# A fused attention and expert kernel: the mixing steps of the last two pairs, the order of the last copies, and the place of the gates

## The chip, the cores and the metric

The kernel runs on one core of one Trainium2 chip. The metric is the device time of the whole program in microseconds, as the median of several runs. The engines are TensorE (PE, with its weight loads PEld), VectorE (DVE), ScalarE (ACT), GpSimd (POOL) and SyncE (SP, which only issues transfers here). They work side by side and are held together by semaphores.

## The reference

Three layers, one behind the other, all in fp32:

```
attention, B=4 batches, H=8 heads, S=576 rows, D=64:
  scores = q @ k.T / 8, causal;  local = softmax(scores) @ v
  phi(x) = elu(x) + 1
  mem    = phi(q) @ M_prev / (phi(q) @ z_prev + 1e-6)
  out    = g * mem + (1 - g) * local,   g = sigmoid(beta) by head
x = out as [2304, 512]
expert layer, 8 experts, F=1024:
  e = argmax(x @ w_gate); gate_w = softmax(x @ w_gate)[e]
  eom = sigmoid(x @ w_output_gate)[e]
  x = gate_w * eom * (relu(x @ w1[e]) @ w2[e])
last layer, 2048 wide:
  h = x @ w_in;  out = (h - tanh(h)) @ w_out
```

## The kernel before, in words

**Attention.** Two heads make a pair; there are NP = 16 pairs (4 to a batch), numbered n from 0. The 576 rows of a pair are QT = 5 steps i of 128 rows (the last has 64). Step m = 5n + i. All engines walk the same two loops, `for n in range(NP + 2)` and `for i in range(QT)`, written out without a loop on the chip, and each has its own order of helpers in the body. For a step, PE computes the scores (`score`), DVE the row maximum (`top`), ACT the exponentials (`exps`), PE turns them (`turn`), and DVE and ACT copy the turned halves to SBUF (`move_a`, `move_b`).

When a pair's five steps are turned, its value products follow one pass later: `average` writes the result for rows 128 to 575 into the PSUM bank `average` (`o_ps[0]`), and `average_first` that for the first 128 into the last quarter of the bank `mix` (`o_ps[1]`, also called `m_ps`). DVE (`move_first`, L880) and ACT (`move_av`, L626) copy both to `ot_sb`. Then come five mixing steps. In `back(n, i)` PE writes phi(q) times M and z, and the turned average, into one bank; in `mix(n, i)` DVE scales both parts to `mixed` (two buffers) with three operations (L897, L900, L905); in `add(n, i)` POOL adds them into `x_sb` (L499) and raises `x_ok`. `phis(n)` on DVE (L911) makes phi(q), `weights_l(n)` (L886 to L891) the sums of the softmax. The banks of the mixing steps are `o_ps[1]`, `o_ps[0]`, `o_ps[1]`, `o_ps[0]`, `o_ps[1]` for i = 0 to 4, so `back` waits from step 2 on for the mix two steps before, and `average` of the next pair waits for `mixed_dve` at 5n - 1, `average_first` at 5n.

**Routing.** When the four pairs of a batch are done, PE turns its `x_sb` (`turn_x`, L1216), ACT copies it (`xlt`), PE makes the logits (`logit`, L1223), DVE picks the expert (`take_logits`, `pick`), PE counts the ranks (`count`), DVE makes row numbers (`place_rows`, `rows_of`), and POOL scatters the rows into `x_sorted` (`scatter`, L506). For batches 0 to 2 this lies inside the passes of the following batch. For the last batch it follows the attention: PE turns step 0 in pass n = 16 between `back(15, 2)` and `back(15, 3)`, step 1 behind `back(15, 3)`, the others behind the loop.

POOL's queue is in order. At pass 16 it does `add(14, 4)`, three scatters of batch 2, then `add(15, 0)` to `add(15, 3)`, at pass 17 `add(15, 4)`, then the five scatters of batch 3.

Behind the routing of the last batch DVE writes how many rows each expert has, and SP and ACT fill unused rows with zeros (`fill`, four each, on their queues; ACT's stand ahead of its `route_exps(B - 1, B)`, L652 and L653). DVE computes the slot table (L1033 to L1061, `r_table`), then waits for ACT's exponentials (`r_exp`), runs `gates_of`, eight operations that make each token's gate (L1012 to L1019), and the corrections L1065 to L1071, and raises `r_tails`. POOL waits for `r_tails` and then makes the low parts of the expert weights, in halves of a unit (L538, `part_lo`); a unit is one expert's w1 or w2. PE meanwhile does 60 idle products (L1172) and then works through 25 slots of 128 rows: `turn_in`, `up` (L1398 to L1400), `turn_hid` (L1420), `down` (L1411 to L1413). `up` of a slot waits for both low halves of its expert's w1. `up` of the next slot is issued ahead of `down` of this one.

In the timelines PE instructions carry the bank's name as their output: `scores`, `turned`, `average`, `mix`, `average` also for the expert layer's results.

Of the kernel before, what the change touches and what calls it, by code (L numbers as in the profile page):

```python
# [8 lines left out]
ALU = mybir.AluOpType  # L9
AX = mybir.AxisListType  # L10

P = 128
B, H, S, D = 4, 8, 576, 64
PAIRS = H // 2
QT = -(-S // P)
NP = B * PAIRS
# [43 lines left out]
def build(nc, qt, qt2, kt2, v, mz, beta, wgo, w1, w2, w_in, w_out, out):  # L60
    ctx = ExitStack()
    with ctx:
# [20 lines left out]
        ident = sb("ident", [P, P], F32)  # L83
# [140 lines left out]
        o_ps = [bank("average"), bank("mix")]  # L224
        m_ps = o_ps[1]

        def mix_ps(i):
            return o_ps[0 if i in (1, 3) else 1]

        def mix4(i):  # L230
            return mix_ps(i)[:, 0:4 * (D + 1)].rearrange("p (a d) -> p a d", a=4)


        c_pool, c_pool2, c_dve, c_dma, c_gate = sem("c_pool"), sem("c_pool2"), sem("c_dve"), sem("c_dma"), sem("c_gate")
# [40 lines left out]
            return [o_ps[0], o_ps[1], t_ps[0]][r]  # L275

        VM = 4 * 16
        last_banks = [s_ps[0][0], s_ps[0][1], s_ps[1][0], s_ps[1][1], o_ps[0]]

        def ring_at(k):  # L280
            return RING - 1 - k % RING
# [547 lines left out]
        def _(dve):  # L829
# [52 lines left out]
            def weights_l(n):  # L882

                p, last = n % 2, QT - 1
                dve.wait_ge(exped, 2 * (n + 1) * QT)
                dve.tensor_copy(sums[0:D, p, last, 1:2], sums[D:P, p, last, 0:1]).then_inc(wts_l, 1)  # L886
                dve.wait_ge(wts_l, 3 * n + 1)
                dve.scalar_tensor_tensor(wts[:, p, :, 0:2], sums[:, p, :, :], 1e-9, inv_l[:, n % PAIRS, :, :], ALU.add, ALU.mult
                                         ).then_inc(wts_l, 1)
                dve.wait_ge(wts_l, 3 * n + 2)  # L890
                dve.reciprocal(wts[:, p, :, 0:2], wts[:, p, :, 0:2]).then_inc(wts_l, 1)  # L891

            def mix(n, i):

                t, p, R = n * QT + i, n % 2, rows(i)
                dve.wait_ge(mixed_pe, t + 1)
                dve.scalar_tensor_tensor(wts[0:R, p, i, 2:4], mix4(i)[0:R, 2:4, D], 1e-6, inv_g[0:R, n % PAIRS, :], ALU.add, ALU.mult  # L897
                                         ).then_inc(wts_step, 1)
                dve.wait_ge(wts_step, 2 * t + 1)
                dve.reciprocal(wts[0:R, p, i, 2:4], wts[0:R, p, i, 2:4]).then_inc(wts_step, 1)  # L900
                dve.wait_ge(wts_step, 2 * t + 2)
                dve.wait_ge(wts_l, 3 * n + 3)
                if t >= 2:
                    dve.wait_ge(x_ok, t - 1)
                dve.tensor_tensor(mixed[0:R, t % 2, :, :], mix4(i)[0:R, :, 0:D], wts[0:R, p, i, :, None].to_broadcast([R, 4, D]),  # L905
                                  ALU.mult).then_inc(mixed_dve, 1)

            def phis(n):
# [64 lines left out]
            for n in range(NP + 2):  # L973
                b, half = divmod(n, PAIRS)
                b -= 1
                for i in range(QT):
                    m = n * QT + i
                    if 0 <= b < B - 1 and i == 3 and half == 2:
                        pick(b)
                    if 0 <= b < B - 1 and i == 3 and half == 3:  # L980
                        rows_of(b)
                        count_so_far(b)
                    if m + 1 < NP * QT:
                        top(m + 1)
                    if 0 <= b < B - 1 and i == 2 and half == 2:
                        take_logits(b, m_ps, LOGITS)
                    if 0 <= b < B - 1 and i == 2 and half == 3:
                        place_rows(b, m_ps, RANKS)
                    if i == 0 and n >= 2:
                        mix(n - 2, QT - 1)  # L990
                    if i == 1 and 1 <= n <= NP:
                        move_first(n - 1)
                    if i == 3 and 1 <= n <= NP:
                        mix(n - 1, 0)
                    if i == 4 and 1 <= n <= NP:
                        mix(n - 1, 2)
                    if n < NP:
                        move_a(m)
                    if i == 3 and n < NP:
                        phis(n)  # L1000
                    if i == 3 and 1 <= n <= NP:
                        mix(n - 1, 1)
                    if i == 4 and 1 <= n <= NP:
                        mix(n - 1, 3)
                    if i == 4 and n < NP:
                        weights_l(n)

            def gates_of(a, z):

                a, z = a * QT, z * QT  # L1010
                sum_e, sum_b = sum_g[:, 0, a:z], sum_g[:, 1, a:z]
                rs(dve.tensor_reduce(sum_e, r_e[:, a:z, :], AX.X, ALU.add))  # L1012
                rs(dve.tensor_scalar(sum_e, sum_e, 1e-9, None, ALU.add))
                rs(dve.reciprocal(sum_e, sum_e))
                rs(dve.tensor_scalar(r_b[:, a:z, :], r_b[:, a:z, :], 1.0, None, ALU.add))
                rs(dve.reciprocal(r_b[:, a:z, :], r_b[:, a:z, :]))
                rs(dve.tensor_tensor(r_b[:, a:z, :], r_b[:, a:z, :], hot[:, a + 1:z + 1, :], ALU.mult))
                rs(dve.tensor_reduce(sum_b, r_b[:, a:z, :], AX.X, ALU.add))
                rs(dve.tensor_tensor(gate[:, a:z], sum_e, sum_b, ALU.mult))  # L1019

            dve.wait_ge(r_exp, 2)
            gates_of(0, B - 1)
            take_logits(B - 1, t_ps[1], 0)
            pick(B - 1)
            place_rows(B - 1, t_ps[0], 0)
# [34 lines left out]
            dve.tensor_scalar(ups[:, :], end_e, 2.0, None, ALU.mult)  # L1060
            dve.tensor_scalar(ends[:, :], end_e, 1.0, None, ALU.add).then_inc(r_table, 1)  # L1061
            dve.wait_ge(r_exp, 4)
            gates_of(B - 1, B)
            wide = [P, TILES, E]
            rs(dve.tensor_tensor(hot2[:, :, :], hot[:, 1:TILES + 1, :], gap_e[:, None, :].to_broadcast(wide), ALU.mult))  # L1065
            rs(dve.tensor_reduce(row_f[:, 1, :], hot2[:, :, :], AX.X, ALU.add))
# [97 lines left out]
        def _(pe):  # L1164
            pe.sem_inc(down_done, 1)
            pe.sem_inc(x_turned, XIN)
            mm = pe.matmul
# [105 lines left out]
            def average(n, js):  # L1273

                p = n % 2
                if js[0] == 0:
                    pe.wait_ge(v_in[p], (n // 2 + 1) * VM)
                    pe.wait_ge(moved_a, (n + 1) * QT)
                    pe.wait_ge(moved_b, (n + 1) * QT)
                    if n:  # L1280
                        pe.wait_ge(mixed_dve, n * QT - 1)
                for j in js:
                    for h in range(2):
                        if j == QT - 1:
                            last = mm(o_ps[0][h * D:(h + 1) * D, S - P - D:S - P], v_sb[0:D, p, j, h * D:(h + 1) * D],
                                      pt_last[0:D, p, h, :], start=False, stop=True)
                        else:
                            a = max(P, j * P)
                            last = mm(o_ps[0][h * D:(h + 1) * D, a - P:S - P], v_sb[:, p, j, h * D:(h + 1) * D],  # L1289
                                      pt[:, p, h, j, a:S], start=j == 0, stop=False)  # L1290
                if js[-1] == QT - 1:
                    last.then_inc(av_done, 1)

            def average_first(n):

                p = n % 2
                if n:
                    pe.wait_ge(mixed_dve, n * QT)
                for h in range(2):
                    last = mm(m_ps[h * D:(h + 1) * D, 512 - P:512], v_sb[:, p, 0, h * D:(h + 1) * D], pt[:, p, h, 0, 0:P],  # L1300
                              start=True, stop=True)
                last.then_inc(first_done, 1)

            def back(n, i):

                t, p, R = n * QT + i, n % 2, rows(i)
                if i == 0:
                    pe.wait_ge(phi_ok, n + 1)
                    pe.wait_ge(first_moved, n + 1)
                else:  # L1310
                    pe.wait_ge(av_moved, n + 1)
                    if i >= 2:
                        pe.wait_ge(mixed_dve, t - 1)
                mm(mix_ps(i)[0:R, 2 * (D + 1):4 * (D + 1)], phi[:, p, i * P:i * P + R],
                   mz_sb[:, p, :, :].rearrange("p h d -> p (h d)"), start=True, stop=True)
                pe.transpose(mix4(i)[0:R, 0:2, 0:D], ot_sb[:, i * P:i * P + R], ident[:, :]).then_inc(mixed_pe, 1)

            score(0)
            for n in range(NP + 2):
# [3 lines left out]
                for i in range(QT):  # L1323
# [27 lines left out]
                            back(n - 1, 2)  # L1351
                    if n < NP:
                        turn(m)
                    if n == NP and i == 4:
                        turn_x((B - 1) * QT, last_banks[0])
                    if 1 <= n <= NP:
                        if i == 0:
                            average(n - 1, [0])
# [2 lines left out]
                        if i == 4:  # L1361
                            back(n - 1, 3)
                    if n == NP and i == 4:
                        turn_x((B - 1) * QT + 1, last_banks[1])
                    if routed and half == 0 and i == 4:
                        turn_x(b * QT, s_ps[(m + 1) % 2][1])
                        turn_x(b * QT + 1, s_ps[m % 2][1])
# [2 lines left out]
                    if routed and half == 1 and i == 4:  # L1370
                        pe.wait_ge(xl_act, b * QT + 3)
                        turn_x(b * QT + 3, s_ps[(m + 1) % 2][1])
                        turn_x(b * QT + 4, s_ps[m % 2][1])

            for i in range(QT):
                if i + 2 < QT:
                    turn_x((B - 1) * QT + i + 2, last_banks[i + 2])
                pe.wait_ge(xl_act, (B - 1) * QT + i + 1)
                logit(i, i % 4, t_ps[1], i * 2 * E).then_inc(logit_ok, 1)
# [153 lines left out]
```

## Time and profile before

| | |
|---|---|
| median of 3 runs | 1031.01 us (1029.05 to 1031.02) |
| profiled execution | 1033.97 us |
| its span in the trace | 1032.1 us |
| mean granted clock of PE | 0.982 of full |
| attention and routing of batches | about 0 to 285 us |
| expert slots | about 300 to 590 us |
| last layer | to the end |

The profile is of one execution. A time in it is counted from the start of the span; an engine's row gives the start and the duration, and in brackets how long the engine had stood idle before, and which engine and line released it ("issue" where the trace shows no releaser). A chain of waits is followed backwards from the last instruction. The column for the granted clock gives PE's clock as a share of 2.4 GHz; 0.50 is 1.2 GHz. The rows themselves stand in a section of their own below.

### The profile page before, as it was taken

The page shows a single profiled execution, that of the slowest core. Times are in us where ns is not written, and L with a number is a line of the kernel's source. Part 1 is how long each engine was busy: PE and PEld are TensorE (multiplying, and loading weights), DVE is VectorE, ACT ScalarE, POOL GpSimd, SP SyncE. Part 2 cuts the span into 40 slices and gives each one's busy share as a digit, 9 for nine tenths or more (in the row PEclk, how much of TensorE's full clock was granted, in tenths as well). Part 3 has the DMA queues.
Part 4 walks back from the last instruction along what each step waited for, and adds up shares of the span by engine and source line. Part 5 has one row for each costly group of instructions (what it writes and reads, how often), then busy time and mean ns, then how long its engine had stood idle before and what let it go on. Part 6 is the DMA issues. An engine that isn't in the chain of part 4 may idle for free.

```text
span 1032.1 us, 16788 instructions
## 1 busy us (share of the span) xinstructions
PE 998.1 (97%) x5474; PEld 821.3 (80%) x5475; DVE 649.1 (63%) x1244; ACT 501.9 (49%) x1043; POOL 468.8 (45%) x332
## 2 busy tenths in 40 slices
PE   6999999899899999999999999999999999999998
PEld 3667667676647888888888879999999999999997
DVE  4687686867544444444444448777777777777764
ACT  5777677686224211022112046556565555555553
POOL 3565587685379933047536137332232322322221
PEclk8999999999889999999999999999999999999999
DMA  9465566531378433146473211010010010100000
GB/s 210 120 164 161 156 191 173 145 108 39 128 250 295 175 123 125 48 150 220 169 273 133 71 41 32 1 31 32 1 62 1 13 50 1 31 31 1 32 1 31
DMA packets 51009, 103.66 MB, mean 100 GB/s; under 512 B 7424, under 2 KB 16640, under 8 KB 50432
## 3 DMA queue, kind: packets, MB, share of 16 engines
q1 hardware_dynamic: 34176, 55.96, 18.8%
q10 hardware_dynamic: 13856, 37.42, 10.2%
q0 software_dynamic: 2912, 9.44, 3.0%
q8 instruction: 37, 0.61, 0.2%
q14 instruction: 28, 0.23, 0.1%
HBM read 82.62 MB, written 20.19 MB: 100 GB/s over the span
## 4 chain that ended last, share of the span: by engine, by line
PE 84%; DVE 10%; issue 2%; POOL 2%; DMA 1%; ACT 1%; ACTq 0%; SPq 0%; DVEq 0%
PE scores L1457 6%; PE scores L1459 6%; PE scores L1458 6%; PE average L1413 4%; PE average L1412 4%; PE average L1411 4%; PE scores L1400 4%; PE scores L1398 4%; PE scores L1399 4%; PE average L1289 4%; PE average L1474 2%; PE scores L1193 2%; PE mix L1475 2%; PE turned L1474 2%; PE average L1475 2%; PE turned L1475 2%
## 5 line engine op out<-in xcount | busy, mean ns | idle before, releaser
L575 POOL TENSOR_TENSOR g_lo<-g,g_hi 128x384 fp32r<-128x384 f32 x96 | 97.9, 1020 | 273.7 <-ACT g_hi L784 273.1
L538 POOL TENSOR_TENSOR ring<-ring 128x2048 fp32r<-128x2048 f32 x30 | 137.4, 4610 | 104.6 <-ACT ring L723 100.8
L723 ACT ACTIVATE ring<-ring 128x2048 fp32r<-128x2048 f32 x30 | 55.7, 1907 | 178.5 <-PE scores L1400 81.7
L1457 PE MATMUL scores<-yt_hi,w_in_hi 128*128 128x384 f32 x384 | 130.9, 341 | 1.7 <-DVE yt_lo L1145 1.7
L1459 PE MATMUL scores<-yt_hi,w_in_lo 128*128 128x384 f32 x384 | 129.3, 337 | 0.0
L1458 PE MATMUL scores<-yt_lo,w_in_hi 128*128 128x384 f32 x384 | 128.8, 335 | 0.0
L774 ACT ACTIVATE sq<-scores 128x384 f32<-128x384 f32 x96 | 47.2, 491 | 163.8 <-PE scores L1459 163.8
L1137 DVE COPY_PREDICATED ser<-big,th 128x384 f32<-128x384 int32 x96 | 119.0, 1240 | 3.3
L1132 DVE TENSOR_TENSOR ser<-ser,sq 128x384 f32<-128x384 f32 x96 | 55.9, 582 | 95.8 <-ACT ser L777 95.8
L601 ACT ACTIVATE prob<-scores,nmx 128x128 f32<-128x128 f32 (+3 forms) x128 | 66.4, 525 | 46.5 <-DVE nmx L862 41.2
L1398 PE MATMUL scores<-ring,xt_hi 128*128 x200 | 80.9, 404 | 3.6 <-POOL ring L538 1.8
L1101 DVE COPY y_sb<-average 128x512 f32<-128x512 f32 x25 | 17.3, 692 | 101.2 <-PE average L1413 101.2
L1411 PE MATMUL average<-ring,hidt_hi 128*128 x200 | 80.0, 400 | 0.6 <-DVE hidt_lo L1095 0.6
L1400 PE MATMUL scores<-ring,xt_lo 128*128 x200 | 78.8, 394 | 0.0
L1399 PE MATMUL scores<-ring,xt_hi 128*128 x200 | 78.8, 394 | 0.0
L1413 PE MATMUL average<-ring,hidt_lo 128*128 x200 | 78.4, 392 | 0.0
L1412 PE MATMUL average<-ring,hidt_hi 128*128 x200 | 78.2, 391 | 0.0
L1086 DVE TENSOR_SCALAR hid<-scores 128x512 f32<-128x512 f32 x50 | 34.6, 692 | 69.2 <-PE scores L1400 69.2
L1457 PEld LDWEIGHTS scores<-yt_hi,w_in_hi 128*128 128x128 f32 x384 | 72.2, 188 | 5.2 <-DVE yt_lo L1145 2.0
L1458 PEld LDWEIGHTS scores<-yt_lo,w_in_hi 128*128 128x128 f32 x384 | 72.2, 188 | 3.1
L1459 PEld LDWEIGHTS scores<-yt_hi,w_in_lo 128*128 128x128 f32 x384 | 72.0, 188 | 0.0
L862 DVE TENSOR_REDUCE nmx<-scores 128x2 f32<-128x256 f32 (+1 forms) x64 | 51.9, 810 | 25.2 <-PE scores L1196 23.7
(259 smaller groups left out, 2510.9 us busy)
## 6 DMA issues: line engine op xcount, KB each, us to landing
ring<-in_w ACTq DMA_DIRECT2D x13, 2048.0 KB, 9.0
q_sb<-in_qt SPq DMA_DIRECT2D x46, 288.0 KB, 4.3
k_sb<-in_kt SPq DMA_DIRECT2D x32, 288.0 KB, 4.2
xin<-x_sorted SPq DMA_DIRECT2D x27, 256.0 KB, 2.9
y_sorted<-y_sb SPq DMA_DIRECT2D x25, 256.0 KB, 2.2
v_sb<-in_v SPq DMA_DIRECT2D x16, 256.0 KB, 2.8
ring<-in_w SPq DMA_DIRECT2D x8, 512.0 KB, 4.1
w_out_sb<-in_w_out ACTq DMA_DIRECT2D x1, 4096.0 KB, 16.1
```

What stands on the lines that cost most here:

```text
L538: pool.tensor_tensor(ring[:, ring_at(k), 1, part], ring[:, ring_at(k), 1, part].bitcast(F32), ring[:, ring_at(k), 0, part].bitcast(F32), A ...
L575: pool.tensor_tensor(g_lo[:, t % GRING, :], g32[:, t % 2, :], g_hi[:, t % GRING, :].bitcast(F32), ALU.subtract).then_inc(g_lo_ok, 1)
L1137: dve.copy_predicated(ser[:, t % 2, :], big[:, t % 2, :].bitcast(I32), th[:, t % 2, :]).then_inc(f_step, 1)
L1398: mm(s_ps[0][j][:, :], xt_hi[:, c, :], h, start=c == 0, stop=False)
L1399: mm(s_ps[0][j][:, :], xt_hi[:, c, :], l, start=False, stop=False)
L1400: last = mm(s_ps[0][j][:, :], xt_lo[:, c, :], h, start=False, stop=c == CD - 1)
L1411: mm(o_ps[0][:, :], hidt_hi[:, c, :], h, start=c == 0, stop=False)
L1412: mm(o_ps[0][:, :], hidt_hi[:, c, :], l, start=False, stop=False)
L1413: last = mm(o_ps[0][:, :], hidt_lo[:, c, :], h, start=False, stop=c == CF - 1)
L1457: mm(ff_h(t), w_h, yt_hi[:, j % 2, c, :], start=c == 0, stop=False)
L1458: mm(ff_h(t), w_h, yt_lo[:, j % 2, c, :], start=False, stop=False)
L1459: last = mm(ff_h(t), w_l, yt_hi[:, j % 2, c, :], start=False, stop=c == CD - 1)
```

## The change

Four things are done to the last two pairs, 14 and 15, and to what follows them.

1. Each of their mixing steps has a PSUM bank of its own (`late_banks`), three of them banks of the scores, which are done by then. `back` of pair 14 no longer waits for earlier mixes, `back` of pair 15 only for the mix of pair 14 that used its bank. The banks for the last batch's turned rows (`last_banks`) are chosen anew to fit.
2. `average` of pair 15 waits for the first two mixing steps of pair 14, not for four, and `average_first` of pair 15 for none.
3. DVE's order in pass 15: the copy of the last turned rows (`move_a`) stands ahead of `phis(15)` and of the mixes 2 to 4 of pair 14; `move_first(15)` and `mix(14, 4)` move from pass 16 to the end of pass 15. On PE, `turn_x` of step 0 of the last batch moves behind `back(15, 3)`, and that of step 1 behind the loop, behind `back(15, 4)`.
4. The gates of batches 0 to 2 are no longer computed ahead of `take_logits` of the last batch but with its own, behind the slot table: one set of eight operations for 20 tiles in place of a set for 15 and one for 5.

```diff
+        late_banks = [o_ps[1], o_ps[0], s_ps[0][0], s_ps[0][1], s_ps[1][0]]
+
-        def mix_ps(i):
+        def mix_ps(n, i):
+            if n >= NP - 2:
+                return late_banks[i]
             return o_ps[0 if i in (1, 3) else 1]
...
-        last_banks = [s_ps[0][0], s_ps[0][1], s_ps[1][0], s_ps[1][1], o_ps[0]]
+        last_banks = [s_ps[1][1], t_ps[0], o_ps[1], o_ps[0], s_ps[0][0]]
...
@@ DVE, the loop of the passes @@
-                    if i == 0 and n >= 2:
+                    if i == 0 and n >= 2 and n != NP:
                         mix(n - 2, QT - 1)
-                    if i == 1 and 1 <= n <= NP:
+                    if i == 1 and 1 <= n < NP:
                         move_first(n - 1)
                     if i == 3 and 1 <= n <= NP:
                         mix(n - 1, 0)
-                    if i == 4 and 1 <= n <= NP:
+                    if i == 4 and 1 <= n <= NP and n != NP - 1:
                         mix(n - 1, 2)
                     if n < NP:
                         move_a(m)
-                    if i == 3 and n < NP:
+                    if n < NP and i == (3 if n < NP - 1 else 4):
                         phis(n)
                     if i == 3 and 1 <= n <= NP:
                         mix(n - 1, 1)
+                    if i == 4 and n == NP - 1:
+                        mix(n - 1, 2)
                     if i == 4 and 1 <= n <= NP:
                         mix(n - 1, 3)
+                    if i == 4 and n == NP - 1:
+                        move_first(n)
                     if i == 4 and n < NP:
                         weights_l(n)
+                    if i == 4 and n == NP - 1:
+                        mix(n - 1, QT - 1)
...
-            dve.wait_ge(r_exp, 2)
-            gates_of(0, B - 1)
             take_logits(B - 1, t_ps[1], 0)
...
             dve.wait_ge(r_exp, 4)
-            gates_of(B - 1, B)
+            gates_of(0, B)
...
@@ PE, average and average_first @@
-                    if n:
+                    if n == NP - 1:
+                        pe.wait_ge(mixed_dve, (n - 1) * QT + 2)
+                    elif n:
                         pe.wait_ge(mixed_dve, n * QT - 1)
...
-                if n:
+                if 0 < n < NP - 1:
                     pe.wait_ge(mixed_dve, n * QT)
...
@@ PE, back @@
-                    if i >= 2:
+                    if i >= 2 and n < NP - 2:
                         pe.wait_ge(mixed_dve, t - 1)
+                    if i >= 2 and n == NP - 1:
+                        pe.wait_ge(mixed_dve, t - QT + 1)
...
@@ PE, the loop of the passes @@
                     if n < NP:
                         turn(m)
-                    if n == NP and i == 4:
-                        turn_x((B - 1) * QT, last_banks[0])
...
                         if i == 4:
                             back(n - 1, 3)
                     if n == NP and i == 4:
-                        turn_x((B - 1) * QT + 1, last_banks[1])
+                        turn_x((B - 1) * QT, last_banks[0])
...
+            turn_x((B - 1) * QT + 1, last_banks[1])
             for i in range(QT):
```

## Rows read from the trace of the kernel before

**Rows 1.** The page, section 1: busy time of each engine.
```profile
PE 998.1 (97%) x5474; PEld 821.3 (80%) x5475; DVE 649.1 (63%) x1244; ACT 501.9 (49%) x1043; POOL 468.8 (45%) x332
```

**Rows 2.** Waits of PE, 283 to 330: total us, times, longest us.
```profile
PE scores L1398 <- POOL ring L538: 1.8, 1, 1.8
PE scores L1398 <- DVE xt_lo L1081: 1.7, 1, 1.7
...
PE turned L1387 <- DMA xin<-x_sorted: 0.8, 1, 0.8
```

**Rows 3.** Chain of waits, 276 to 330: start, duration, what.
```profile
294.98 18.09 POOL ring L538 x4
313.20 0.50 PE scores L1398
```

**Rows 4.** Timeline of DVE: start, duration, instruction, idle before and releaser.
```profile
275.85 0.26 DVE L1012 TENSOR_REDUCE sum_g<-r_e 128x15 f32<-128x120 f32 x1
...
278.63 0.17 DVE L1019 TENSOR_TENSOR gate<-sum_g 128x15 f32<-128x15 f32 x1
282.23 0.24 DVE L930 COPY L<-turned 128x80 f32<-128x80 f32 x1 [3.43 <-PE turned L1223]
...
291.60 0.20 DVE L1012 TENSOR_REDUCE sum_g<-r_e 128x5 f32<-128x40 f32 x1 [0.75 <-ACT r_b L653]
...
293.38 0.17 DVE L1019 TENSOR_TENSOR gate<-sum_g 128x5 f32<-128x5 f32 x1
```

**Rows 5.** Timeline of DVE, 261 to 267.
```profile
261.04 0.68 DVE L874 COPY pt<-turned 128x512 f32<-128x512 f32 x1
261.63 0.75 DVE L911 SCALAR_TENSOR_TENSOR phi<-qexp,q_sb 128x576 f32<-128x576 f32 x1
...
262.69 0.42 DVE L905 TENSOR_TENSOR mixed<-average,wts 128x256 f32<-128x256 f32 x1
...
263.41 0.42 DVE L905 TENSOR_TENSOR mixed<-mix,wts 128x256 f32<-128x256 f32 x1
...
265.19 0.15 DVE L886 COPY sums<-sums 64x1 f32<-64x1 f32 x1
...
266.04 0.42 DVE L905 TENSOR_TENSOR mixed<-mix,wts 64x256 f32<-64x256 f32 x1
```

**Rows 6.** Timeline of PE, 260 to 270.
```profile
261.87 0.63 PE L1258 MATMUL turned<-ident,prob 128*128 128x128 f32 x4
...
265.30 0.97 PE L1289 MATMUL average<-pt,v_sb 128*64 128x448 f32 x4 [0.69 <-DVE mixed L905]
```

**Rows 7.** Chain of waits, 255 to 300: PE's tail.
```profile
271.61 1.00 PE scores L1216 x4
272.61 0.43 PE average L1314 x2
273.05 0.21 PE average L1316
```

**Rows 8.** Timeline of POOL, 260 to 275.
```profile
263.19 0.46 POOL L499 TENSOR_TENSOR x_sb<-mixed 128x128 f32<-128x128 f32 x1 [1.53 <-DVE mixed L905]
...
267.60 0.99 POOL L506 DMA_INDIRECT x_sorted<-x_sb,row_u  x1 [0.16 <-issue]
...
271.09 0.87 POOL L499 TENSOR_TENSOR x_sb<-mixed 128x128 f32<-128x128 f32 x2
```

**Rows 9.** Timeline of PE: 24 logit products of an earlier pass, and the last 24.
```profile
240.82 2.53 PE L1223 MATMUL mix<-wgo_sb,xlt 128*128 128x16 f32 x24
...
278.05 4.08 PE L1223 MATMUL turned<-wgo_sb,xlt 128*128 128x16 f32 x24
```

**Rows 10.** Busy time of PE, PEld, DVE, ACT, POOL by stretch; then granted clock, DMA.
```profile
272.00:275.00 3.00, 3.00 (x14) 2.33 (x13) 0.86 (x4) 1.20 (x2) 0.92 (x2) 0.50 0.06 14
302.60:305.70 3.10, 3.07 (x7) 2.49 (x8) 0.00 (x0) 0.00 (x0) 3.10 (x2) 0.50 0.98 327
313.20:316.00 2.80, 2.80 (x12) 2.33 (x13) 1.15 (x2) 1.50 (x1) 2.80 (x1) 1.00 0.56 222
```

More of the change, by code:

```diff
@@ L225, in build, with mix4 @@
         m_ps = o_ps[1]
-        def mix_ps(i):
+        late_banks = [o_ps[1], o_ps[0], s_ps[0][0], s_ps[0][1], s_ps[1][0]]
+        def mix_ps(n, i):
+            if n >= NP - 2:
+                return late_banks[i]
             return o_ps[0 if i in (1, 3) else 1]
-        def mix4(i):
-            return mix_ps(i)[:, 0:4 * (D + 1)].rearrange("p (a d) -> p a d", a=4)
+        def mix4(n, i):
+            return mix_ps(n, i)[:, 0:4 * (D + 1)].rearrange("p (a d) -> p a d", a=4)
         c_pool, c_pool2, c_dve, c_dma, c_gate = sem("c_pool"), sem("c_pool2"), sem("c_dve"), sem("c_dma"), sem("c_gate")
@@ L896, in mix @@
                 dve.wait_ge(mixed_pe, t + 1)
-                dve.scalar_tensor_tensor(wts[0:R, p, i, 2:4], mix4(i)[0:R, 2:4, D], 1e-6, inv_g[0:R, n % PAIRS, :], ALU.add, ALU.mult
+                dve.scalar_tensor_tensor(wts[0:R, p, i, 2:4], mix4(n, i)[0:R, 2:4, D], 1e-6, inv_g[0:R, n % PAIRS, :], ALU.add, ALU.mult
                                          ).then_inc(wts_step, 1)
@@ L904, in mix @@
                     dve.wait_ge(x_ok, t - 1)
-                dve.tensor_tensor(mixed[0:R, t % 2, :, :], mix4(i)[0:R, :, 0:D], wts[0:R, p, i, :, None].to_broadcast([R, 4, D]),
+                dve.tensor_tensor(mixed[0:R, t % 2, :, :], mix4(n, i)[0:R, :, 0:D], wts[0:R, p, i, :, None].to_broadcast([R, 4, D]),
                                   ALU.mult).then_inc(mixed_dve, 1)
@@ L1311, in back @@
                     pe.wait_ge(av_moved, n + 1)
-                    if i >= 2:
+                    if i >= 2 and n < NP - 2:
                         pe.wait_ge(mixed_dve, t - 1)
-                mm(mix_ps(i)[0:R, 2 * (D + 1):4 * (D + 1)], phi[:, p, i * P:i * P + R],
+                    if i >= 2 and n == NP - 1:
+                        pe.wait_ge(mixed_dve, t - QT + 1)
+                mm(mix_ps(n, i)[0:R, 2 * (D + 1):4 * (D + 1)], phi[:, p, i * P:i * P + R],
                    mz_sb[:, p, :, :].rearrange("p h d -> p (h d)"), start=True, stop=True)
-                pe.transpose(mix4(i)[0:R, 0:2, 0:D], ot_sb[:, i * P:i * P + R], ident[:, :]).then_inc(mixed_pe, 1)
+                pe.transpose(mix4(n, i)[0:R, 0:2, 0:D], ot_sb[:, i * P:i * P + R], ident[:, :]).then_inc(mixed_pe, 1)
             score(0)
```

## The prediction

> **What bounds the kernel now.** I read the page first, then the waits of TensorE (PE) in the stretches around the change, then the chain of waits backwards from the wait found there, and last the timelines of POOL, PE and VectorE (DVE), link by link. PE is busy 998.1 of 1032.1 us [rows 1]: a change counts only where it moves a place at which PE stands still. Between 283 and 330 us the longest wait of PE is that for POOL at line L1398 [rows 2], up to 313.20, and the view of waits lists none for PE from there to 550 us. All that follows is work in a row; what moves the restart at 313.20 moves the end one for one, as far as the trace reaches.
>
> What ends at 313.20? The first slot of the second expert needs both halves of that expert's first weight unit as low parts. POOL makes four such halves in a row, 18.09 us from 294.98 [rows 3], and it can't begin before DVE's `r_tails` (the wait stands in front of the loop over the units). Behind `r_tails` the code and the chain read: tails, row corrections, the second `gates_of`, from 291.60, which waited for ScalarE's (ACT's) exponentials [rows 4]; these stand in ACT's queue behind its four zero fills; the fills wait for the count of rows, that for the choice of expert, and that for PE's last logits, which DVE takes at 282.23 [rows 4]. PE's own work had ended 1.85 us before 313.20, so POOL is the bound by something under that.
>
> The diff touches two links of this chain: PE's tail of the attention, up to 282.23, and `gates_of`.
>
> **The last two pairs: what gets earlier.** Before, DVE's order behind the copy of turned rows at 261.04 is phi(15), mix(14,1) (its product at 262.69), mix(14,2) (263.41), the copy of the last turned rows, mix(14,3), the sums (265.19), mix(14,4) (266.04) [rows 5], and PE's value products wait for it until 265.30 [rows 6]. Now that copy stands ahead of phi and of the mixes 2 to 4. mix(14,1) follows the copy of 261.04 directly, so it starts where phi did, at 261.63, and its product 0.39 behind that, at 262.02: 0.67 us earlier [rows 5]. PE's last transposes end at 262.50 [rows 6]; they wait for the copy of 261.04, which doesn't move. So the last copy runs from 262.54 to 263.22 (0.68, as the one at 261.04), and PE, which no longer waits in back(14,3) and back(14,4), starts the value products at about 263.45: 1.85 us earlier. The averages behind them lose a short wait as well, and end at about 266.7. Some two microseconds are won on PE.
>
> **Where they go.** The next thing on PE that counts is turn_x(15), at 271.61 [rows 7]. It waits for `x_ok`, POOL's add(15,0), which starts at 271.09 [rows 8]. POOL works in order: add(14,4), three scatters of the batch before, add(15,0). From add(14,1) at 263.19 to 271.09 POOL waits for nobody: 7.90 us of its own work. Begun 0.67 earlier it would end 0.67 earlier, but add(14,4) also needs mix(14,4), and DVE now does that one last. My sum for DVE: last copy 262.54, phi 263.13, the product of mix(14,2) at 264.19, that of mix(14,3) 0.72 behind it (262.69 to 263.41 before) at 264.91, `move_first` at 265.26 (about 0.29, a quarter of the columns of the copy at 261.04 and the same start), the sums at 265.55, and 0.85 behind these (265.19 to 266.04 before) the product of mix(14,4), 266.40 to 266.82 [rows 5]. So add(14,4) starts at 266.90 and the scatters about 0.61 behind it (an add of 0.46 and 0.16 of issue), at 267.51, where before they began at 267.60 [rows 8]; add(15,0) starts at 271.00. **x_ok comes 0.09 us earlier.** Bounds: 0.67 earlier, if DVE is never late; 0.6 later, if the order costs phi's 0.67 more than I gave it. I take 0.09, the step by step sum.
>
> From there PE has a string of work without a gap: turn_x, back(15,3), turn_x, back(15,4), turn_x, logits and so on, from 271.61 to 282.13 [rows 7, 9]. back(15,3) held PE for 0.43 + 0.21 = 0.64 us of it [rows 7], and is now done before the wait for x_ok; back(15,4) isn't, it stands behind turn_x(15). mix(15,4) then ends near 273.9 and the last add near 274.4, before the fifth turn_x asks (it was issued some six us behind the first). The five new banks give no new wait, since the former reader of each is done before its x_ok. **The logits end 0.64 + 0.09 = 0.73 us earlier**; bounds: 0.37 (the same work at twice the clock), and rival (b) above.
>
> **Gates behind the slot table: what gets later.** The first set, for 15 tiles, ran from 275.85 to 278.80 while DVE had nothing to do: it stood idle for 3.43 us behind it [rows 4]. Taking it from there gives nothing. The second, for 5 tiles, ran from 291.60 to 293.55, on the chain, and becomes one set for 20. 2.95 us for 120 elements of the wide tile and 1.95 for 40 are 1.00 for 80, so 160 elements are 2.95 + 0.50 = 3.45: **1.50 us more** than the 5 tiles took. Bounds: 1.00 (only the step from 5 to 15 tiles) and 2.95 (the sets simply add up). I take 1.50, since all eight operations are the same with longer rows. Being free earlier doesn't help DVE: it had waited 0.75 us for ACT's exponentials there [rows 4], and now nothing of the set can start before them.
>
> **The sum.** POOL starts its halves at 294.98 - 0.73 + 1.50 = 295.75, and PE restarts at 313.20 + 0.77 = 313.97. The profiled execution took 1033.97 us (span 1032.10 and 1.87 around it): it would take 1034.7. It lies 2.96 us above the median of the three runs, 1031.01; to that I add the same 0.77: **1031.8 us**. A measurement of this kernel tells about 0.2%, 2.06 us, from no change, so this is no change.
>
> **Rivals.** (a) *Slower: the clock falls while PE waits.* PE's wait in front of slot 1 grows from 1.85 to 1.85 + 0.73 + 0.77 = 3.35 us. After the 1.85 PE worked on at 2.4 GHz (granted 1.00) [rows 10]. But behind two waits of 0.84 and 1.71 [rows 2], with one short burst between them, the first slot ran at 0.50, that is 1.2 GHz, from 302.6 to about 305.7 [rows 10]: 3.1 us at half the rate, 1.55 lost. 0.77 + 1.55 = +2.3, 1033.3. It decides where the wait is longer than those two together, 2.55 us, and 3.35 is. Against it: the three runs of before lie 2 us apart, so some may pay this fall already, and those would pay only 0.77 more.
>
> The Trainium skill, TensorE: Matmul & The Clock Gate, section "What's actually happening", says that the monitor of the clock runs freely and isn't reset by a kernel's start. By that rule one and the same wait may cost a fall in one execution and none in the next; the page gives no sum for this place, and one profile of before can't show it.
>
> (b) *Faster: the clock stays up in the tail.* From 272 to 275 it was granted 0.50 [rows 10], where full clock would give back 1.5 of 3.0 us; and the last 24 logit products took 4.08 us, against 2.53 for 24 in an earlier pass [rows 9]: 1.55. Together 0.77 - 1.5 - 1.55 = -2.3, 1028.7. For it: PE's averages come without gaps. Against: PE now stands still from about 268.8 to 271.5, where before it had the backs to do.
>
> (c) *The gates are hidden*, because POOL isn't what PE waits for: then only -0.73 stays, 1030.3. Against: the wait for POOL in [rows 2].
>
> **Chances.** Forecast 0.45, (a) 0.30, (b) 0.13, (c) 0.12. With runs that lie 2 us apart I put 0.40 of the forecast, 0.08 of (a), 0.03 of (b) and 0.10 of (c) within 0.2%: 0.61. Slower: 0.22 of (a) and 0.03 of the forecast, 0.25. Faster: 0.10 of (b) and 0.02 each of (c) and the forecast, 0.14. The range reaches from 1029.3 (toward (b), which it leaves out) to 1033.9 ((a), and the later x_ok of the bounds): 8 in 10.
>
> **What would show it.** In the profile after: the value products of pair 15 start near 263.5; add(15,0) stays near 271.0 and turn_x(15) near 271.5, with PE idle for about 2.7 us before it; the last logits are taken near 281.5; there is one set of gates, of 3.4 to 3.5 us; POOL's first half starts near 295.75 and PE is back near 314.0, released by POOL. If add(15,0) comes over 0.5 us earlier, my sum of DVE's order is wrong; if the wide set takes under 2.5 us, the price of the gates; if POOL doesn't release PE there, the bound itself; if PE's first products behind that wait run at 0.50, it is rival (a).

## The result, and the profile after

The changed kernel takes **1035.57 us** as the median of nine executions in two sessions (1034.81 to 1037.20), the kernel before 1030.5 us as the median of 68 (1028.63 to 1034.16). The ratio is 1.0054 with a 95% interval of 1.0036 to 1.0071 in the first comparison, and 1.0057 (1.0039 to 1.0075) in the second: **5 us slower**, where no change was forecast and the range ended at 1033.9. One of the nine executions of a kernel shown further down (the gates alone) took 1944.7 us, for no reason on record; the ratios leave it out.

The page of the changed kernel, section 1, against [rows 1]:

```profile
span 1033.1 us, 16776 instructions
...
PE 996.5 (96%) x5474; PEld 819.9 (79%) x5475; DVE 647.9 (63%) x1236; ACT 502.0 (49%) x1043; POOL 468.9 (45%) x332
```

This execution took 1034.94 us, only 0.97 more than the profiled execution of before. That one, at 1033.97, was an unusually long one: 66 of the 68 timed executions are shorter. So two single profiles laid side by side hide most of the loss; it has to be read stage by stage, and over several profiles.

This execution came to the copy of the fourth turned rows (before at 261.04, [rows 5]) already at 258.54. That isn't the change, which begins behind it: the same point lies between 258.4 and 261.2 in all fourteen profiles (one of each kernel and rerun in this document), early and late with either order. Distances from it are what to compare. DVE, POOL and PE after:

```profile
258.54 0.68 DVE L878 COPY pt<-turned 128x512 f32<-128x512 f32 x1
...
260.04 0.69 DVE L875 COPY pt<-turned 128x512 f32<-128x512 f32 x1
...
264.19 0.42 DVE L909 TENSOR_TENSOR mixed<-scores,wts 64x256 f32<-64x256 f32 x1
...
279.08 0.24 DVE L934 COPY L<-turned 128x80 f32<-128x80 f32 x1 [7.09 <-PE turned L1231]
...
288.47 0.32 DVE L1022 TENSOR_REDUCE sum_g<-r_e 128x20 f32<-128x160 f32 x1 [0.76 <-issue]
...
291.53 0.18 DVE L1029 TENSOR_TENSOR gate<-sum_g 128x20 f32<-128x20 f32 x1
```

```profile
264.68 0.45 POOL L503 TENSOR_TENSOR x_sb<-mixed 64x128 f32<-64x128 f32 x1 [0.34 <-DVE mixed L909]
265.29 0.99 POOL L510 DMA_INDIRECT x_sorted<-x_sb,row_u  x1 [0.16 <-issue]
...
268.78 0.87 POOL L503 TENSOR_TENSOR x_sb<-mixed 128x128 f32<-128x128 f32 x2
```

```profile
260.97 0.97 PE L1299 MATMUL average<-pt,v_sb 128*64 128x448 f32 x4
...
269.30 0.89 PE L1224 MATMUL scores<-ident,x_sb 128*128 128x128 f32 x4 [3.27 <-POOL x_sb L503]
...
275.39 3.66 PE L1231 MATMUL turned<-wgo_sb,xlt 128*128 128x16 f32 x24
```

The value products start 2.43 us behind the copy, where before it was 4.26. But POOL's add(15,0) starts 10.24 behind it and not 10.05 ([rows 5, 8]), because the three scatters still stand in front of it, and PE, done early, now stands still for 3.27 us. The last logits are taken 20.54 behind the copy instead of 21.19; POOL's first low half follows them by 14.06 instead of 12.75 ([rows 3, 4]). The waits of PE from 262 to 325, against [rows 2], and the chain at the restart, against [rows 3]:

```profile
PE scores L1409 <- POOL ring L542: 3.3, 1, 3.3
PE scores L1224 <- POOL x_sb L503: 3.3, 1, 3.3
PE turned L1398 <- DMA xin<-x_sorted: 1.8, 1, 1.8
PE scores L1409 <- DVE xt_lo L1089: 1.7, 1, 1.7
```

```profile
293.14 18.09 POOL ring L542 x4
311.36 0.79 PE scores L1409
312.15 0.43 PE scores L1410
```

PE waits for the same POOL as before, 3.3 us instead of 1.85, and behind the wait a product comes every 0.43 us, where before one came every 0.23. The stretches, against [rows 10] (length; busy time and, in brackets, instructions of PE, PEld, DVE, ACT, POOL; then the granted clock, the DMA share and GB/s):

```profile
265.90:269.30 3.40, 0.13 (x3) 0.00 (x1) 0.55 (x3) 0.00 (x0) 2.77 (x5) 1.00 0.41 154
269.30:279.10 9.80, 9.75 (x63) 8.84 (x63) 1.82 (x8) 2.77 (x5) 1.71 (x4) 0.69 0.63 219
311.40:317.40 6.00, 6.00 (x14) 4.76 (x15) 0.52 (x1) 3.72 (x2) 6.00 (x2) 0.50 0.48 148
```

From the restart to the end of the span it is 1033.1 - 311.36 = 721.74 us; before, 1032.1 - 313.20 = 718.9. The same products, 2.84 us longer: about six microseconds at 1.2 GHz.

The tail between turn_x and the last logits, in three stretches, first of before and then of the changed kernel:

```profile
271.90:275.00 3.10, 3.10 (x15) 2.43 (x14) 0.96 (x4) 1.20 (x2) 0.98 (x3) 0.50 0.12 25
275.10:278.70 3.60, 3.60 (x34) 3.51 (x33) 3.26 (x11) 1.58 (x3) 0.45 (x1) 0.97 0.26 58
278.80:282.10 3.30, 3.30 (x20) 3.18 (x19) 0.00 (x1) 0.00 (x0) 0.00 (x0) 0.50 1.02 408
```

```profile
269.50:272.70 3.20, 3.20 (x16) 2.54 (x15) 1.69 (x7) 1.20 (x2) 1.51 (x4) 0.51 0.13 27
272.90:276.40 3.50, 3.50 (x32) 3.40 (x33) 0.00 (x0) 1.58 (x3) 0.00 (x0) 0.99 0.78 252
276.50:279.00 2.50, 2.50 (x16) 2.40 (x15) 0.00 (x0) 0.00 (x0) 0.00 (x0) 0.50 1.02 415
```

The clock is down, up and down again in both, so this pair of profiles shows no loss in the tail. The loss there shows only in other executions.

### The profile page after: what moved, and what is told of

It reads as the page before. It is cut to its first block, busy times and chain, and to the rows that moved or that the text cites. A ratio compares the mean times of both kernels' runs of the same rounds, so it can differ in the third digit from the quotient of the medians.

```text
span 1033.1 us, 16776 instructions
## 1 busy us (share of the span) xinstructions
PE 996.5 (96%) x5474; PEld 819.9 (79%) x5475; DVE 647.9 (63%) x1236; ACT 502.0 (49%) x1043; POOL 468.9 (45%) x332
## 4 chain that ended last, share of the span: by engine, by line
PE 84%; DVE 10%; POOL 2%; issue 2%; DMA 1%; ACT 0%; SPq 0%; DVEq 0%; ACTq 0%
PE scores L1468 6%; PE scores L1470 6%; PE scores L1469 6%; PE average L1424 4%; PE average L1423 4%; PE average L1422 4%; PE scores L1409 4%; PE scores L1410 4%; PE scores L1411 4%; PE average L1299 4%; PE scores L1201 2%; PE average L1485 2%; PE mix L1486 2%; PE turned L1485 2%; PE average L1486 2%; PE turned L1486 2%
## 5 line engine op out<-in xcount | busy, mean ns | idle before, releaser
L1409 PE MATMUL scores<-ring,xt_hi 128*128 x200 | 81.9, 409 | 5.0 <-POOL ring L542 3.3
L1410 PE MATMUL scores<-ring,xt_hi 128*128 x200 | 80.0, 400 | 0.0
```

What stands on the lines that cost most here:

```text
L1409: mm(s_ps[0][j][:, :], xt_hi[:, c, :], h, start=c == 0, stop=False)
L1410: mm(s_ps[0][j][:, :], xt_hi[:, c, :], l, start=False, stop=False)
```

## The experiments

Three distances carry the argument. *Tail*: from the copy named above to the last logits. *Gates*: from there to POOL's first low half. *End*: from PE's restart with expert 1 to the end of the span.

**The changed kernel again.**

> The changed kernel once more, for a second profile and a time beside the others. Theory 1: 4 to 5.5 us slower than before; PE's wait for POOL 3.3 us with the clock down behind it for one or two stretches of three microseconds. Theory 2 (the first times were chance of the machine): within 1.5 us of the kernel before.

Measured: 1036.48 us, 1.0057 (1.0039 to 1.0075). Tail 20.47, gates 13.97, wait for POOL 4.99 us, end 720.25. Theory 1 holds in kind. Here the clock was down behind the restart for about three microseconds.

**The kernel before, twice more.**

> The kernel before, once more, for a second profile: the first profiled execution took 1033.97 us, 3.9 above the median of 20 timed ones. Theory 3 (the tail's clock is what the change loses): in a usual execution PE's clock is up in the logits, turn_x of step 0 to take_logits lasts about 7.7 us as in the run with the gates alone, not 10.6, and the first slot of expert 1 starts near 310. Theory 1 (gates and the clock behind PE's wait for POOL alone): the tail lasts 10 us here too, and only the stretch behind slot 1's start is shorter than in the changed kernel.

> The kernel before, a third profile. The same as for the one before it: theory 3 says a tail of about 7.7 us from turn_x of step 0 to take_logits in most executions, theory 1 about 10 us.

Measured: 1031.50 and 1031.08 us, one execution each. The tail is not one number: turn_x to the logits took 10.59 us in the first and 7.82 in the second. Here is the tail and then the restart, first of the one and then of the other:

```profile
269.10:279.70 10.60, 10.49 (x66) 9.58 (x66) 4.54 (x15) 2.77 (x5) 1.75 (x4) 0.67 0.51 171
310.70:316.70 6.00, 6.00 (x29) 5.00 (x30) 2.23 (x5) 4.63 (x3) 6.00 (x2) 1.00 0.44 153
```

```profile
270.80:278.60 7.80, 7.69 (x67) 7.11 (x66) 4.96 (x19) 2.77 (x5) 1.81 (x4) 0.94 0.45 141
310.30:316.30 6.00, 6.00 (x29) 5.03 (x30) 2.57 (x5) 4.43 (x3) 6.00 (x2) 1.00 0.40 127
```

The same 66 or 67 products ran at a mean clock of 0.67 in the one and 0.94 in the other. In the second the clock had been down earlier, in the value products (granted 0.50 from 264.3 to 267.1), and was up again for turn_x. The whole tail was 21.19, 21.14 and 18.74 in three profiles of before, and the end 718.9, 719.03 and 718.9: the clock never falls at the restart there. Of theory 3 half is right: the fast tail occurs, but in one of three, not in most.

**The gates alone, in the kernel before.**

```diff
-            dve.wait_ge(r_exp, 2)
-            gates_of(0, B - 1)
...
-            gates_of(B - 1, B)
+            gates_of(0, B)
```

> The kernel before with one part of the change alone: one set of gates for 20 tiles behind the slot table. Theory 1: POOL starts 1.4 us later, PE waits about 3.3 us and not 1.85, the clock falls behind the wait and stays down for 3 to 6 us: 1.4 + 1.5 to 2.9 = 2.9 to 4.3 us slower than before, 1033 to 1034.4. Theory 2: no change, within 1 us of 1030.1.

Measured: 1032.81 us, ratio 1.0029 (1.0013 to 1.0045). Tail 18.67, gates 13.99 (12.72 to 12.78 before), wait for POOL 3.49 us, end 720.58. So the gates cost 2.3 us over the median of all executions of before, or 3.0 by the ratio to those of the same session; theory 1 had 2.9 to 4.3. Of this 1.2 is the gates themselves, and the end is 1.7 us longer, by the clock behind the longer wait:

```profile
269.40:277.10 7.70, 7.67 (x68) 7.05 (x66) 2.40 (x10) 2.77 (x5) 1.82 (x4) 0.96 0.44 136
309.30:315.30 6.00, 5.98 (x19) 4.80 (x20) 0.69 (x1) 3.83 (x3) 6.00 (x2) 0.72 0.51 137
```

**The changed kernel with the gates in their old place.**

```diff
+            dve.wait_ge(r_exp, 2)
+            gates_of(0, B - 1)
             take_logits(B - 1, t_ps[1], 0)
...
-            gates_of(0, B)
+            gates_of(B - 1, B)
```

> The changed kernel with the gates of batches 0 to 2 computed where they were before, ahead of the last logits; all else as changed. Theory 1 (gates on the chain, and the clock): POOL's first low half starts about 1.4 us earlier against take_logits, PE's wait in front of the first slot of expert 1 shrinks from 3.3 to about 1.8 us, and the clock stays up behind it. Against the changed kernel 1.4 + 2.8 = 4.2 us faster, about 1031.3; against the kernel before 0.7 us faster to 1 us slower. Theory 2 (the loss is in the attention's tail or before it, not in the gates): stays within 1 us of the changed kernel, near 1035.5, 5 us slower than before.

Measured: 1034.61 us, 1.0038 (1.0023 to 1.0053). Theory 1 as put there fell: only 1.0 us came back, and 4 us stay without the gates. Tail 20.61, gates 12.69 (the 1.3 us did come back), but the wait for POOL was 3.83 and the end 720.56. PE had run the first slot at full clock (its first product took 0.49 us, against 0.79 in the kernel before), was ready earlier, and waited longer; the fall then hit the restart, where nothing hides it. So the new order alone loses 4 us and the gates alone 2.3 to 3.0, and together they lose 5: the fall at the restart stands in both (ends of 720.56 and 720.58) and is paid once. The larger part lies in the new order, which led to theory 3.

**PE's new wait in the tail filled.** On top of the kernel just shown:

```diff
                     if n == NP and i == 4:
+                        idle_products(last_banks[0], 14)
                         turn_x((B - 1) * QT, last_banks[0])
```

> The changed kernel with the gates back in their old place, and 14 idle products (3.0 us at full clock, nothing computed) on PE between back(15,3) and turn_x of step 0, where it stood idle for 3.3 us. Theory 3: the clock doesn't fall there, turn_x to take_logits lasts 7.5 us and not 9.9; 2.4 us faster than with the gates back alone (1034.6), about 1032.2. Theory 1: the wait filled changes nothing by itself, 1034.6.

Measured: 1030.16 us, 0.9997 (0.9987 to 1.0007): 4.45 us faster than without the 14 products, where theory 3 had 2.4, and level with before. They compute nothing. PE's timeline, and the stretches of tail and restart:

```profile
265.86 3.19 PE L1182 MATMUL scores<-onesb 128*128 128x512 bf16 x14
269.30 0.66 PE L1226 MATMUL scores<-ident,x_sb 128*128 128x128 f32 x4 [0.26 <-issue]
...
273.83 2.53 PE L1233 MATMUL turned<-wgo_sb,xlt 128*128 128x16 f32 x24
```

```profile
269.30:276.50 7.20, 7.06 (x63) 6.50 (x63) 4.47 (x16) 2.67 (x5) 1.72 (x4) 1.00 0.57 176
309.40:315.40 6.00, 5.96 (x29) 4.99 (x29) 2.56 (x5) 4.64 (x3) 6.00 (x2) 1.00 0.41 131
```

turn_x starts at 269.30 as in the first profile of the changed kernel, and the same 63 products take 7.2 us instead of 9.8. So with the new order it was PE's standing still, and not the work, that made the tail slow. This is the tail's share, though, and not all of the 4.45 us: the tail is 17.93, 2.7 shorter, and the end 718.96, 1.6 shorter. The end gained because PE came to the restart later. It had waited 1.97 us for its rows and begun the first slot at the low clock (its first product took 0.79 us), so it waited only 1.39 us in front of expert 1 and kept its clock behind that.

**The wait in front of expert 1 filled.** 13 products in the changed kernel, then 18; 18 also with the gates back.

```diff
             turn_hid(0)
+            idle_products(t_ps[1][:, :], 13)
```

> The changed kernel with 13 idle products of 512 columns (0.213 us each at full clock, 2.8 us in all) put between turn_hid(0) and the loop over the slots, where PE waits 3.3 us for POOL. They compute nothing that is used. Theory 1 (the clock is the larger half of the loss): the first slot of expert 1 runs at 2.4 GHz, 2.8 us faster than the changed kernel, about 1032.7; the restart itself doesn't move. Theory 2 (the clock at this place costs nothing that isn't paid before too): within 0.5 us of the changed kernel, or slower by what the idle products overrun.

> The changed kernel with 18 idle products (3.8 us) in the wait in front of the first slot of expert 1. 13 of them left a wait of 2.3 us in the profile and the clock still fell. Theory: now the rest of the wait is 0 to 1.3 us, the clock stays up and the restart to the end takes 718.9 us, not 720.3 to 721.7: 1033.2 to 1034, 1.5 to 2.4 faster than the changed kernel. Rival (the products' own overrun, or a fall that comes in any case): 1034.5 or more.

> The changed kernel with the gates in their old place and 18 idle products in the same wait. It parts the 4.0 to 4.5 us by which that kernel is slower than before: what this fill gives is the clock's fall at the restart (theory: 1.7 us, 1032.9), what stays is the tail (theory: 2 to 2.5 us above before, from PE's 3.3 us of standing still ahead of turn_x). Rival (the tail is all of it): no change, 1034.6.

Measured: 1034.23 (1.0035, 1.0021 to 1.0050), 1033.11 (1.0030, 1.0019 to 1.0041) and 1033.13 us (1.0024, 1.0015 to 1.0034). With 13 a wait of 2.31 us was left and the clock still fell (end 720.47); with 18 it didn't. The restart of the third, and the clock behind it:

```profile
309.08 4.05 PE L1182 MATMUL turned<-onesb 128*128 128x512 bf16 x18
312.82 0.54 PE L1411 MATMUL scores<-ring,xt_hi 128*128 x1
```

```profile
269.30:281.90 12.60, 12.45 (x63) 11.62 (x63) 4.49 (x16) 2.77 (x5) 1.71 (x4) 0.52 0.51 178
...
313.00:319.00 6.00, 6.00 (x30) 5.00 (x29) 1.07 (x2) 4.43 (x3) 6.00 (x2) 1.00 0.46 148
```

The end is 1034.2 - 315.08 = 719.1 in the second and 1031.8 - 312.82 = 719.0 in the third. By the medians the fill is worth 2.5 us in the changed kernel (1035.57 to 1033.11) and 1.5 with the gates back (1034.61 to 1033.13), near what was expected. The intervals overlap, so these sizes are rough, that of the 13 products (1.3 us, 2.8 expected) above all. In the second the idle products also ended 1.3 us behind POOL's last half and held the restart back by that.

The first line shows the rest: here the tail took 12.6 us at 0.52. But for its idle products this third kernel differs from before by the new order alone; its gates (12.72) and its end are as before. What it still loses by its twelve executions, 1.0024 or 2.5 us (1.5 to 3.5), is left to the tail. Of six profiles of kernels with the new order, POOL's queue as it was and no fill in the tail, three had a tail of 20.5 to 20.6 and three (these three, whose products come only behind the tail) one of 23.1 to 23.3.

**The scatters moved, in three kernels.** POOL's three scatters of batch 2 go from ahead of add(15,0) to behind add(15,4):

```diff
-                if n == NP:
-                    for i in range(2, QT):
-                        scatter(B - 2, i)
...
+            for i in range(2, QT):
+                scatter(B - 2, i)
             for i in range(QT):
                 scatter(B - 1, i)
```

> The changed kernel with the gates back, and POOL's three scatters of batch 2 moved from ahead of add(15,0) to behind add(15,4). Theory (POOL's queue takes what the new order wins): x_ok of step 0 comes about 3 us earlier, turn_x follows back(15,3) with a wait under 1 us, the clock stays up, and the logits end 3 to 5 us earlier than with the gates back alone: 1030 to 1031.5. Rival (something else holds the tail, such as DVE's mixes or the last scatters' transfers): under 1 us faster, 1034.

> The kernel before with POOL's three scatters of batch 2 moved behind add(15,4), nothing else. Theory (the new order wins 2 us on PE, and POOL's queue and then the clock take them back): here POOL held turn_x of step 0 for only 0.7 us, so 0.7 to 1.5 us faster than before, 1029.5, and the kernel with both (1025.2) owes 4 us or more to the new order. Rival (the scatters were the whole matter, the new order is worth nothing even with POOL free): near 1025.5.

> The changed kernel, its gates behind the slot table as they are, with the three scatters moved behind add(15,4). Against the same kernel with the gates in their old place (1025.2): POOL starts 1.3 us later, PE's wait in front of the first slot of expert 1 grows from 1.9 to 3.2 us or more, and the clock falls behind it for 1.5 to 2.8 us: 1028 to 1029.3. Rival (the gates' delay alone): 1026.5, with 718.9 us from the restart to the end.

Measured: with the new order and the old gates **1025.22 us**, 0.9957 (0.9944 to 0.9970); in the kernel before 1030.94, 0.9998 (0.9987 to 1.0009), no change in the median; in the changed kernel 1027.84, 0.9973 (0.9963 to 0.9984). POOL and PE of the first:

```profile
264.77 0.46 POOL L503 TENSOR_TENSOR x_sb<-mixed 64x128 f32<-64x128 f32 x1 [0.35 <-DVE mixed L908]
265.57 0.46 POOL L503 TENSOR_TENSOR x_sb<-mixed 128x128 f32<-128x128 f32 x1 [0.34 <-DVE mixed L908]
...
268.53 0.45 POOL L503 TENSOR_TENSOR x_sb<-mixed 64x128 f32<-64x128 f32 x1 [0.24 <-DVE mixed L908]
269.13 0.98 POOL L510 DMA_INDIRECT x_sorted<-x_sb,row_u  x1 [0.16 <-issue]
```

```profile
266.09 0.66 PE L1225 MATMUL scores<-ident,x_sb 128*128 128x128 f32 x4
...
270.68 2.53 PE L1232 MATMUL turned<-wgo_sb,xlt 128*128 128x16 f32 x24
```

add(15,0) starts 0.80 us behind add(14,4), where in the changed kernel the scatters made it 4.1 (264.68 to 268.78 above). turn_x follows with no wait, the 24 logit products run at full clock, and the tail is 14.97 us: 5.6 less than with the scatters in front. The time is 9.4 us less, where 3 to 5 was expected. Between the two profiles it is 5.6 in the tail, 1.7 in the end (718.86), and 2.1 only because this execution came to the copy earlier. Against the kernel before it is 5.3 us (1030.5 to 1025.2), and 5.7 against that kernel with its scatters moved.

In the kernel before neither the 0.7 to 1.5 us of the theory came, nor the 5 of its rival. The median hides two kinds of executions, though: three of the twelve took 1027.4 to 1027.7 us, less than all 68 of before, at a mean granted clock of 0.988, the other nine 1030.4 to 1032.3 at 0.982 to 0.985. The profiled one is of the longer kind. POOL and a stretch of it:

```profile
271.58 0.46 POOL L499 TENSOR_TENSOR x_sb<-mixed 128x128 f32<-128x128 f32 x1 [4.03 <-DVE mixed L904]
```

```profile
265.40:268.80 3.40, 3.37 (x12) 1.48 (x14) 1.32 (x7) 0.00 (x0) 1.96 (x4) 0.51 0.41 154
```

With the old order add(15,0) now waits 4.03 us for DVE's mix, which follows PE's value products, and those ran at half clock. It starts 10.42 behind the copy, no earlier than with the scatters in front. So in such an execution the old order hides what the freed queue would win, as the queue hides what the new order wins. What an execution of the shorter kind gains, and where, is not shown, for none was profiled.

The gates behind the table cost 2.6 us here as well (1025.22 to 1027.84), 1.3 by themselves (gates 14.00) and up to 1.75 by the clock, with a wait for POOL of 3.49 and an end of 720.61; the rival that left the clock out said 1026.5. The profiled execution of this kernel, at 1030.94, is the longest of its seven by 2.9 us. Its tail is 16.24, because the last 24 logit products took 4.21 us, though PE had waited for nothing since the value products:

```profile
272.70:275.90 3.20, 3.20 (x20) 3.16 (x19) 0.00 (x0) 0.00 (x0) 0.94 (x2) 0.50 0.92 337
```

So PE's standing still is one way to a slow tail, not the only one.

## Why the prediction was wrong

- **That POOL's low halves set PE's restart**: right in nine of the fourteen profiles, the pair compared here among them. In three (the third of before, the kernel before with its scatters moved, and the one with the tail filled) POOL was done first and PE waited 1.38 or 1.39 us for DVE's `xt_lo`, and in two the 18 idle products ended last. So its margin was thinner than the 1.85 us of one profile.
- **The sum for DVE and POOL up to `x_ok`**: right. Value products 2.43 us behind the copy (2.41 forecast); add(15,0) 10.24, against 9.96 forecast and 10.05 before, so 0.19 later and not 0.09 earlier. The three scatters took the two microseconds, as said.
- **"The logits end 0.73 us earlier"**: this is the step that failed. In the pair of profiles it looks right (21.19 to 20.54, 0.65). But it took the tail's clock of one profiled execution for a property of the kernel. Over the profiles the tail is 21.19, 21.14, 18.74 and 18.67 us with the old order, 19.9 in the mean, and 20.54, 20.47, 20.61, 23.25, 23.07 and 23.33 with the new one, 21.9: **2 us later, not 0.7 earlier**. The changed kernel's own two profiles don't show this by themselves; it rests on the quick tail, which came in two of four profiles with the old order (and at 18.75 in that with the scatters moved) and in none of six with the new one, on the slow tails of 23 us, and on the 2.5 us that stay when all but the tail is as before. I had seen that PE would stand still for 2.7 us ahead of turn_x (3.27 measured) and used it only as an argument against rival (b), the gain; I gave no price to the loss. With the wait filled the tail was 17.93 in its one profile, 2.7 us less than without.
- **The gates, 1.50 us more**: right in kind, 1.2 to 1.4 measured; the set took 3.27 us (288.47 to the next operation at 291.74), not 3.45. That it gained nothing to be moved was right too.
- **Rival (a), the clock behind PE's wait in front of expert 1**: it happened in every profile of the changed kernel and of those with one of its halves. The wait was forecast at 3.35 us and measured 3.31, and 4.99 in the second profile. I had tied it to waits above 2.55 us, and one of 2.31 was enough. Its chance of 0.30 was too small, and its price is 1.4 to 2.8 us (1.55 forecast). The forecast left it out of the sum, and it is the second term that is missing there. I held against it that runs of before may pay it already: three of three did not, at this place.
- **The sum**: forecast -0.73 + 1.50 = +0.77. Measured by the means of the profiles, tail +2.0, gates +1.3, end +2.1 (718.9 to 721.74 and 720.25), together +5.4, with 5.1 between the medians. The parts are means of few profiles, and each can be off by a microsecond.

What stays open: why the tail comes in two lengths with the same wait ahead of it, 9.8 and 12.5 us. In the shorter the clock comes back after some three microseconds and falls again in the logits, in the longer it stays down throughout, and the traces show no difference in PE's work before it. Open too is why it falls in the logits when PE has not stood still (in the kernel before, and in the changed kernel with its scatters moved), and what decides whether the kernel before has it down in the value products or behind them.

## What to carry to other kernels

When an engine is made ready earlier but what it waits for isn't, the gain turns into one long wait, and here such waits of PE cost a second time, by the clock behind them. Look in the queue of the engine that releases it for work that can stand behind the released one: here three scatters, worth nothing in the median alone and 5 us together with the new order. And a stage at half clock in one profile is a sample; price a stage at both clocks before using it in a sum.

## What the runs showed of the hardware

Behind PE's wait in front of expert 1 the clock fell to 1.2 GHz in all six profiles in which that wait was 2.31 to 4.99 us (within 0.2 us of the restart in three, 0.5 to 1.5 us behind it in the other three), and stayed at 2.4 GHz in all six in which it was 1.38 to 1.89 us. That is what these runs show of this place, and no rule for others: in the tail it also fell without a wait. In the changed kernel's first profile the first slot, where POOL hides a fall (302.6 to 305.7 before), ran at full clock, and the restart, where nothing does, at the low one. That fall cost 2.84 us, though no more time was spent at the low clock: the mean granted clock was 0.982 before and 0.983 after. With the gates alone both places fell.

Reciprocal on DVE took 0.40, 0.90 and 1.15 us for 40, 120 and 160 elements in a row, 6.25 ns for each further one (0.75 us over 120). The other seven operations of the set grew by 0.5 us together from 40 to 160.
